# A reordered step and front in a three-part fused kernel (windowed attention, rational MLP, soft mixture of experts) on one core

## The reference, cut to what matters

```python
# q, k, v: (4, 8, 768, 64); 8 memory keys and values; chunks of 32 queries,
# each sees 16 positions to the left, its own 32, 8 to the right, and the memory
for each chunk:
    scores = scale * q_c @ k_full.T
    a = exp(scores - max); a = a / (sum(a) + 1e-9)
    out_c = a @ v_full
x = out as (3072, 512)

h = x @ w_in                                  # 512 -> 2048
P = a0 + a1*h + a2*h^2 + a3*h^3
Q = 1 + |b0|*|h| + |b1|*h^2
y = (P / (Q + 1e-6)) @ w_out                  # 2048 -> 512

logits = y @ phi                              # 32 slots
d = softmax over tokens of logits; slot_input = d.T @ y
slot_out = relu(slot_input[e] @ w1[e]) @ w2[e]     # 8 experts, 4 slots each
out = (softmax over slots of logits) @ slot_out
```

## Time and profile before

| | |
|---|---|
| median of 3 executions | 532.05 us (531.46 to 533.24) |
| the profiled execution | 531.5 us, its span 529.7 us |
| PE busy | 508.4 us, 96% of the span |
| DVE busy | 444.1 us, 84% |
| ACT busy | 401.4 us, 76% |
| granted TensorE clock, mean | 0.994 |
| start of h(0,0), h(1,0), h(2,0), h(3,0) | 16.34, 36.47, 54.95, 74.89 us |
| start of h(23,0), the last tile's first block | 437.04 us |
| last quarter of expert weights lands | 513.7 us |

### The profile page before, as it was taken

One profiled execution on the slowest core, in us unless ns is written; L12 is line 12 of the kernel. 1 busy time (PEld: TensorE's weight loads), 2 busy tenths in 40 slices (PEclk: granted clock), 3 DMA queues, 4 the chain that ended last, 5 costly groups with the idle time before them and its releaser, 6 DMA issues.

```text
span 529.7 us, 15871 instructions
## 1 busy us (share of the span) xinstructions
PE 508.4 (96%) x6604; PEld 385.3 (73%) x6604; DVE 444.1 (84%) x824; ACT 401.4 (76%) x775; POOL 0.2 (0%) x4
## 2 busy tenths in 40 slices
PE   8889999999999999999999999999999999999982
PEld 7657777877787787778777877877787777645452
DVE  5797989999999999999999999999999999652143
ACT  1868979888988988898889889888988898612032
POOL 0000000000000000000000000000000000000000
PEclk9999999999999999999999999999999999999997
DMA  8982374244113121312231231223131226999997
GB/s 343 421 316 64 130 257 157 77 173 165 56 62 101 48 96 61 103 43 86 76 86 58 62 101 62 83 61 103 42 100 63 82 82 264 412 409 409 408 410 312
DMA packets 23399, 85.31 MB, mean 161 GB/s; under 512 B 2592, under 2 KB 2720, under 8 KB 21408
## 3 DMA queue, kind: packets, MB, share of 16 engines
q1 hardware_dynamic: 23184, 84.09, 43.5%
q10 hardware_dynamic: 144, 0.20, 0.1%
HBM read 77.99 MB, written 6.29 MB: 159 GB/s over the span
## 4 chain that ended last, share of the span: by engine, by line
PE 87%; DMA 4%; DVE 3%; ACT 2%; issue 2%; SPq 1%; DVEq 0%
PE hb L409 17%; PE hb L411 16%; PE hb L410 16%; PE gb L339 9%; PE sl L456 4%; PE at L339 4%; PE mb L433 4%; PE at L362 3%; PE at L386 3%; DMA place<-w 2%; DMA g<-w_in 2%; PE at L598 1%; PE hb L598 1%; PE mb L441 1%; PE sl L345 1%
## 5 line engine op out<-in xcount | busy, mean ns | idle before, releaser
L409 PE MATMUL hb<-w_hi,x_hi 128*128 128x512 f32 x384 | 162.5, 423 | 0.0
L411 PE MATMUL hb<-w_hi,x_lo 128*128 128x512 f32 x384 | 151.9, 396 | 0.0
L410 PE MATMUL hb<-w_lo,x_hi 128*128 128x512 f32 x384 | 151.3, 394 | 0.0
L715 ACT ACTIVATE hs<-hb 128x512 f32<-128x512 f32 x96 | 57.3, 597 | 49.4 <-PE hb L411 48.1
L411 PEld LDWEIGHTS hb<-w_hi,x_lo 128*128 128x128 f32 x384 | 72.2, 188 | 17.8
L409 PEld LDWEIGHTS hb<-w_hi,x_hi 128*128 128x128 f32 x384 | 72.2, 188 | 14.2 <-issue 0.2
L410 PEld LDWEIGHTS hb<-w_lo,x_hi 128*128 128x128 f32 x384 | 72.5, 189 | 12.0
L928 DVE SCALAR_TENSOR_TENSOR qq<-h,few,ab 128x512 f32<-128x512 f32 x96 | 71.7, 747 | 10.8 <-ACT h L717 10.7
L933 DVE SCALAR_TENSOR_TENSOR tt<-tt,cst,hs 128x512 f32<-128x512 f32 x96 | 72.1, 751 | 3.4
L722 ACT ACTIVATE qq<-qq,few 128x512 f32<-128x512 f32 x96 | 70.2, 731 | 5.7 <-DVE qq L928 4.3
L943 DVE SCALAR_TENSOR_TENSOR g<-tt,cst,qq 128x512 f32<-128x512 f32 x96 | 71.3, 746 | 2.5 <-ACT qq L726 0.5
(11 more groups left out here) (154 smaller groups left out, 543.0 us busy)
## 6 DMA issues: line engine op xcount, KB each, us to landing
place<-w SPq DMA_DIRECT2D x60, 512.0 KB, 10.2
v_in<-v_windows SPq DMA_DIRECT2D x24, 520.0 KB, 3.8
kw<-k_windows SPq DMA_DIRECT2D x24, 512.0 KB, 4.6
qT<-q_t SPq DMA_DIRECT2D x24, 256.0 KB, 2.7
wout<-w_out_t SPq DMA_DIRECT2D x4, 1024.0 KB, 14.3
wout<-w_out SPq DMA_DIRECT2D x4, 1024.0 KB, 6.6
g<-w_in SPq DMA_DIRECT2D x3, 1024.0 KB, 9.2
out_dram<-o_c SPq DMA_DIRECT2D x6, 512.0 KB, 5.6
```

The lines of the kernel that those rows point to most:

```text
L409: mm(o, x_hi[:, p, xs], w_hi[:, f, kd, :], start=kd == 0, stop=False)
L410: mm(o, x_hi[:, p, xs], w_lo[:, f, kd, :], start=False, stop=False)
L411: i = mm(o, x_lo[:, p, xs], w_hi[:, f, kd, :], start=False, stop=kd == KD - 1)
```

## The change

The step functions lose their dynamic form and take n; the steps N and N+1 become a `drain` of its own. What moves:

- PE in a step: p_transposes goes up to directly behind g_transposes 0; g_transposes 2 goes up to directly behind g_transposes 1; attend goes up ahead of block 2 (behind add_quadrants); behind block 2 come g_transposes 3, d_transpose and x_transposes; block 3 is one piece.
- g_transposes 2 writes bank 2 of `at` instead of `gb` and waits for the copy of the P transposes (`pT_sb`); x_transposes waits for the copy of g_transposes 2.
- ACT in a step: softmax_exp goes ahead of the reads of block 0; pT_copy ahead of the inverse of block 0; gT_copy 2 behind gT_copy 1; gT_copy 3 ahead of x_high.
- DVE in a step: softmax_max goes first, then activation(prev, 2), accumulate for tile n-3, activation(prev, 3); o_norm goes ahead of cubic 1.
- The front: the third w_in block is loaded ahead of the second tile's q and k; ACT splits block 1 ahead of the first x_high; w_high and w_low are cut into halves; scores of tile 1 move from ahead of h(0,0) to behind it; step 0 has an order of its own with the first half of block 3 and two `wp_product` ahead of x_transposes. In step 2 `wp_copy` is ACT's first work.

```diff
@@ PE
             def g_transposes(b, t, f):
                 n = b * T + t
                 pe.wait_ge(g_done, FC * n + f + 1)
-                last = isinstance(n, int) and n == N - 1 and f < FC - 1
-                if not last:
-                    need(pe, gT_sb, FC * n + f - (FC - 1 if isinstance(n, int) and n == N - 1 else 0))
+                if n < N - 1 and f != 2:
+                    need(pe, gT_sb, FC * n + min(f, 2))
+                elif n < N - 1:
+                    need(pe, pT_sb, min(n + 3, N))
+                elif f == FC - 1:
+                    pe.wait_ge(gT_sb, FC * n)
...
+            def step(n):
+
+                here, nxt, prev, prev2, nxt2 = (tile(n + o) for o in (0, 1, -1, -2, 2))
+                hidden(*here, 0)
+                if n == 0:
+                    scores(*nxt)
...
                 if prev:
                     g_transposes(*prev, 0)
+                if nxt and n > 0:
+                    p_transposes(*nxt)
+                hidden(*here, 1)
...
                 if prev:
                     g_transposes(*prev, 1)
+                    g_transposes(*prev, 2)
+                if prev2:
                     add_quadrants(*prev2)
+                if n == 0:
                     p_transposes(*nxt)
+                elif nxt:
                     attend(*nxt)
+                hidden(*here, 2)
+                if n == 0:
+                    attend(*nxt)
+                    hidden(*here, 3, range(0, KD // 2))
+                    wp_product(0)
+                    wp_product(1)
                 if prev:
                     g_transposes(*prev, 3)
                 if prev2:
                     d_transpose(*prev2)
                 if nxt:
                     x_transposes(*nxt)
+                hidden(*here, 3, range(KD // 2 if n == 0 else 0, KD))
...
@@ ACT
+                if nxt and n > 0:
+                    softmax_exp(*nxt)
+                hidden_reads(*here, 0)
+                if n == 0:
                     w_high(3)
+                    softmax_exp(*nxt)
...
+                hidden_reads(*here, 2)
...
+                inverse(FC * n + 1, 1)
+                inverse2(FC * n + 1, 1)
+                if prev:
+                    gT_copy(*prev, 3)
                 if nxt:
                     x_high(*nxt)
+                hidden_reads(*here, 3)
+                inverse(FC * n + 2, 0)
+                inverse2(FC * n + 2, 0)
@@ DVE
+                if nxt:
+                    softmax_max(*nxt)
+                if prev:
+                    activation(*prev, 2)
+                if prev3:
+                    accumulate(*prev3)
                 if prev:
                     activation(*prev, 3)
+                cubic(*here, 0)
...
+                activation(*here, 0)
+                if prev2:
                     running_max(*prev2)
+                if nxt and n > 0:
                     o_norm(*nxt)
+                cubic(*here, 1)
                 if prev2:
                     d_copy(*prev2)
...
+                cubic(*here, 2)
                 if nxt:
                     x_low(*nxt)
+                activation(*here, 1)
+                cubic(*here, 3)
```

More of the change, by code:

```diff
@@ L392, in x_transposes @@
                 pe.wait_ge(soft, SOFT * n + SOFT)
+                need(pe, gT_sb, FC * (n - 2) + FC - 1)
                 for hp in range(HP):
@@ L474, in wp_turns @@
                 i.then_inc(wpT_psum, 1)
[L476 to L492, removed]
+            def step(n):
[3 more added lines that the diff above has]
+                    scores(*nxt)
+                if n == 1:
                     wp_product(2)
@@ L546, in step, with drain @@
                     scores(*nxt2)
+            def drain():
+                last, ahead = tile(N - 1), tile(N - 2)
+                g_transposes(*last, 0)
+                g_transposes(*last, 1)
+                add_quadrants(*ahead)
+                pe.wait_ge(h_read, FC * N)
+                spin_drain(B, 0, 1)
+                g_transposes(*last, 2)
+                spin_drain(B, 0, 4)
+                g_transposes(*last, 3)
+                spin_drain(B, 0, 3)
+                logits(*last)
+                d_transpose(*ahead)
+                spin_drain(B, 0, 1)
+                add_quadrants(*last)
+                slots(*ahead)
+                d_transpose(*last)
+                spin_drain(B, 0, 1)
+                slots(*last)
             pe.wait_ge(consts_done, 2)
@@ L557, in _ @@
             x_transposes(0, 0)
[L558 to L568, removed]
+            spin(6, sl, acc)
+            for n in range(N):
+                step(n)
+            drain()
             spin_drain(B, 2, 3)
@@ L764, in wp_copy, with step @@
                   ACT.Copy).then_inc(wp_sb, 1)
[L766 to L779, removed]
+            def step(n):
+                here, nxt, prev, prev2 = (tile(n + o) for o in (0, 1, -1, -2))
+                if n == 2:
+                    wp_copy()
                 if prev:
@@ L794, in step @@
                     gT_copy(*prev, 0)
[L795 to L801, removed]
+                if nxt and n > 0:
+                    pT_copy(*nxt)
+                inverse(FC * n, 0)
+                inverse2(FC * n, 0)
+                hidden_reads(*here, 1)
+                if n == 0:
+                    pT_copy(*nxt)
@@ L802, in step @@
                 if prev:
                     gT_copy(*prev, 1)
-                if nxt:
-                    pT_copy(*nxt)
-                if drain:
                     gT_copy(*prev, 2)
-                    gT_copy(*prev, 3)
                 if prev2:
                     dispatch_exp(*prev2)
-                if here:
-                    hidden_reads(*here, 2)
-                if known and n == 1:
+                hidden_reads(*here, 2)
+                if n == 1:
                     wp_row_copy()
-                if prev and not drain:
-                    gT_copy(*prev, 2)
@@ L830, in w_high, with drain @@
+                inverse(FC * n + 2, 0)
+                inverse2(FC * n + 2, 0)
+            def drain():
+                last, ahead = tile(N - 1), tile(N - 2)
+                part_copy(*ahead)
+                inverse(FC * N - 1, 1)
+                inverse2(FC * N - 1, 1)
+                for f in range(FC):
+                    gT_copy(*last, f)
+                dispatch_exp(*ahead)
+                part_copy(*last)
+                dispatch_exp(*last)
             def w_high(f):
                 act.wait_ge(win_ready[f], 16)
-                A(w_hi[:, f, :, :], w_raw[f], ACT.Copy).then_inc(w_hi_done, 1)
+                for half in range(2):
+                    ks = slice(2 * half, 2 * half + 2)
+                    A(w_hi[:, f, ks, :], w_raw[f][:, ks, :], ACT.Copy).then_inc(w_hi_done, 1)
@@ L971, in accumulate, with step @@
                                        op0=ALU.mult, op1=ALU.add).then_inc(acc_done, 1)
[L974 to L985, removed]
+            def step(n):
+                here, nxt, prev, prev2, prev3 = (tile(n + o) for o in (0, 1, -1, -2, -3))
+                if nxt:
[4 more added lines that the diff above has]
+                    accumulate(*prev3)
@@ L986, in step @@
                 if prev:
                     activation(*prev, 3)
[L988 to L992, removed]
+                cubic(*here, 0)
+                if n == 0:
                     w_low(3)
-                if here:
-                    activation(*here, 0)
-                if prev2 and n <= N:
+                activation(*here, 0)
+                if prev2:
                     running_max(*prev2)
-                if n == N:
-                    accumulate(*tile(-3))
@@ L1011, in step, with drain @@
                     x_low(*nxt)
[L1012 to L1017, removed]
+                activation(*here, 1)
+                cubic(*here, 3)
+            def drain():
+                last, ahead = tile(N - 1), tile(N - 2)
+                activation(*last, 2)
+                activation(*last, 3)
+                running_max(*ahead)
+                accumulate(*tile(N - 3))
+                d_copy(*ahead)
+                running_max(*last)
+                accumulate(*ahead)
+                d_copy(*last)
+                accumulate(*last)
```

105 lines of the change are left out of this document (31 added, 74 removed).

## The result

The changed kernel takes 540.69 us (median of 4 executions, 540.48 to 541.65) against 531.78 us before (4 executions in the same comparison, the three shown above among them): a ratio of 1.0173, 95% interval 1.016 to 1.0185. It is 1.7% slower. The prediction was 540.5 us.

The account below looks back on a forecast made before the run. PE bound the old steps (18.15 us); a three-engine ring of 18.51 would bound the new. Steps and masks 9.9 us later, front 1.2 earlier: 8.7 on 531.5 is 540.2; adjusted to the median, 540.5 us, range 533.5 to 544.0.

Parts of the forecast that it names:

- the one number to forecast: How much earlier or later than 437.04 us h(23,0) starts, taken to move the end equally; forecast 8.7 us later.
- The ring: Chain from p_transposes through PE, ACT and DVE to the next step's p_transposes; 18.51 us, said to set the step.
- PE's own step: A middle step's time on PE alone in the new order: 18.15 to 18.20 us, taken as 18.19.
- The joined block 3: Removing the cut in block 3 on PE: priced at 0, gain of up to 0.1 us a step.
- Masked tiles: Memset ahead of the maximum on DVE adds 0.38 us in seven of the twenty steps: 2.7 us.
- The front: Steps 0 to 2, ahead of h(3,0): 1.2 us gained, bounds 0 and 2.5.
- The three waits forecast for steps 1 and 2: PE waits 0.8 us in step 1, h(2,0) 0.4 for x_low, p_transposes 0.9 in step 2.
- the term I had named as the risk: h(0,0), taken 0.2 us earlier; a later landing of w_in's block 1 would cost here.
- PE did not stay the bound: Rival: p_transposes never waits, steps stay 18.19 us, total 531.7 us, between 529.5 and 533.5; chance 0.17.
- The dependent link: Activation 1 to cubic 3 on DVE, taken as 0.85 us; rival 0.66, giving 536.7 us, chance 0.08.
- g_transposes 2 never waited: Rival of a second wait on PE, for ACT's pT_copy: 0.3 us more a step is 546 us; chance 0.06.
- The tail did not starve: Rival that gates in the drain's weight stream cost once, 1 to 3 us, within the range; no separate chance.

Follow-up runs that it names:

- e5: Changed kernel without the memsets that mask the scores of each batch's first and last tile; 539.12 us, ratio 1.015.
- e3: Changed kernel with x_high ahead of gT_copy 3 and cubic 3's intermediate in its slot of g; 532.82 us, ratio 1.0024.
- e1: Changed kernel with x_high ahead of gT_copy 3 on ACT; 536.44 us, ratio 1.0098.
- e2: Changed kernel with cubic 3's intermediate in g, so its first operation no longer waits for activation 1; 536.43 us, ratio 1.0092.
- e6: Changed kernel with two needless transposes of dT behind slots in every step from 2 on; 542.31 us, ratio 1.0195.
- e7: Kernel before the change with two needless transposes of dT behind slots in each step; 541.44 us, ratio 1.0181.
- e4: Kernel before the change with the new front alone, steps from 1 on as before; 528.47 us, ratio 0.9935.
- e9: Changed kernel with attend, g_transposes 2, block 3's cut, o_norm, gT_copy 2 and x_high back at their old places; 533.84 us, ratio 1.0044.

## Why the prediction was right, point by point

- **What bounds the kernel, and the one number to forecast.** h(23,0) moved by 9.91 us and the median by 8.9. The first expert quarter released by it moved by the same 9.91 (440.13 to 450.04), and so did the last one's landing (513.7 to 523.6). The span moved by 0.9 less, because the six stores at the end landed sooner (median 4.7 us against 5.6). The part from h(23,0) to the end of the span is between 91.5 and 92.7 us over the eleven profiled executions (92.7 before, 91.7 in the changed kernel, 92.6 in e5, 91.5 in e3), and does not follow the edits. That spread, with the 0.19 us at h(3,0), is why e5's time shows only 1.6 of its 2.4 us. One row was read a little wrong: in the earlier trace rows the slice that begins at 437 us has 264 GB/s, and 408 to 412 begins with the next one, which changes nothing in the argument.
- **The ring.** Forecast 18.51 us, measured 18.56. Term by term: p_transposes to block 2 5.39, measured 5.42 (a waiting p_transposes takes 0.41 to 0.42 us to block 1, not 0.39); block 2 to its first read 3.09, measured 3.10; to x_high 3.33, measured 3.32; x_low 0.62, the same; x_low to subtraction 4.67, measured 4.69; to p_transposes 1.41, the same. That the ring, and not PE, is the bound is shown by e1, e2 and e3 (work moved or a wait taken away, PE's work untouched, the time falls by what was computed) and by e6 against e7. The ring's margin over PE, which decides between forecast and rival, was 18.56 against 18.14.
- **PE's own step.** Forecast 18.15 to 18.20, taken 18.19; e6 makes it 18.14. The joined block 3 brought nothing that shows.
- **Masked tiles.** Forecast 7 x 0.38, measured 0.33 in four and 0.38 in three: 2.46 us instead of 2.66. e5 shows it as 2.4.
- **The front.** Forecast 1.2 us, measured 0.84 at h(3,0). The three waits forecast for steps 1 and 2 (0.8, 0.4, 0.9 us) are there, as 0.54, 0.36 and 0.67 by the column in brackets. h(0,0) started 0.15 us later instead of 0.2 earlier: the second block of w_in landed at 13.1 us, x_high came behind it at 15.04, x_low at 15.65. This is the term I had named as the risk. The gain of step 0 was 2.3 us (2.5 forecast), and e4 shows that without the new steps nothing of it is lost later.
- **Cancelling.** The steps lost 10.75 us, not 9.9, and the front gained 0.84, not 1.2; the stores at the end hid 0.9 of it. The forecast also lies 0.25 us under its own sum: 532.05 + 8.7 is 540.75, and so is 540.2 + 0.55. So the time came out within 0.2 us, which is luck; the mechanism was right, but the sum for h(23,0) was 1.2 us short.
- **Rivals.** PE did not stay the bound (e6 shows what that looks like: p_transposes 0.81 us behind exp, and a step that grows with PE's work). The dependent link was 0.85 (e2). g_transposes 2 never waited: PE's waits in the stretch are for exp alone, and it starts 0.43 us behind g_transposes 1. The tail did not starve.

## What to carry to other kernels

When the busiest engine never waits and the next one is near 95%, moving a consumer up is not free: write down the ring from that instruction through every engine back to itself, in start-to-start distances, and compare it with the busiest engine's own step. What is placed between the consumer and the block whose result feeds the ring (here attend and g_transposes 2 ahead of block 2) lengthens it by its full time, 5.42 us against 4.09 in e9, even if the busiest engine's work stays the same. The gain of taking it out ends where another chain becomes the longest: in e9 the step fell by 0.33 us and not by 1.33. And test a change with two parts as two kernels: here the front alone was 0.65% faster and the step cost 2.4% more (1.0173 over 0.9935).

## What was unexpected of the hardware

Two full-array transposes between two tiled groups cost 0.49 us instead of 0.22: leaving and re-entering the tiled form costs about 0.13 us each way here (e7). The Trainium skill (TensorEngine Tiling (Array Packing), Key Properties) names a drain when the tiling mode changes. The runs agree and give the seam a size; what in the engine takes that time they do not tell. In this kernel it speaks for keeping tiled groups together.

A memset on DVE starts only 0.84 us behind an operation of 0.75 us (93.52 to 94.36 above), where other operations follow the same one in 0.66 (149.91 to 150.57), so that it costs more than its own 0.11 us. Why it starts late, no run shows.
